# Running sums of logarithms and angles in a fused attention, expert and feed-forward kernel: exact fp32 products against products of numbers split in two parts

## The reference, cut to what matters

```python
mag = np.sqrt(a_re * a_re + a_im * a_im)
scale = np.minimum(mag, 0.999) / (mag + 1e-06)
a_re_n, a_im_n = (a_re * scale, a_im * scale)
for t in range(S):
    ar, ai = (a_re_n[:, :, t, :, None], a_im_n[:, :, t, :, None])
    new_re = ar * S_re - ai * S_im
    new_im = ar * S_im + ai * S_re
    kv = np.einsum('bhd,bhe->bhde', k[:, :, t], v[:, :, t])
    S_re, S_im = (new_re + kv, new_im)
    y[:, :, t] = np.einsum('bhd,bhde->bhe', q[:, :, t], S_re)
```

## Time and profile before

| what | value |
|---|---|
| median of 3 runs | 857.96 us (855.4 to 858.24) |
| the profiled execution | 854.9 us |
| its span, first to last instruction | 853.1 us |
| granted TensorE clock over the span | 0.996 of full speed |
| PE busy | 834.0 us, 98% |
| DVE, ACT, POOL busy | 362.0, 343.4, 158.8 us |

### The profile page before, as it was taken

How to read it: one execution, slowest core, us unless ns; L and a number is a source line. 1 busy time by engine, 2 the same in 40 slices (tenths; PEclk the granted TensorE clock), 3 DMA queues, 4 the chain that set the end, 5 groups by cost and what they waited for, 6 DMA issues and landing times.

```text
span 853.1 us, 13184 instructions
## 1 busy us (share of the span) xinstructions
PE 834.0 (98%) x5174; PEld 744.4 (87%) x5174; DVE 362.0 (42%) x677; ACT 343.4 (40%) x636; POOL 158.8 (19%) x196
## 2 busy tenths in 40 slices
PE   8899999999998899999999999999999999999997
PEld 6578888888897799999998998999999999999997
DVE  1588888889685333333322222132132132132112
ACT  6888988898653121111113222222222222222221
POOL 3111212622514124456200001001001001001001
PEclk9999999999999899999999999999999999999999
DMA  9999798586433689889600001001001001001001
GB/s 170 153 179 273 95 141 118 99 122 86 119 135 131 183 224 240 211 229 260 220 1 1 1 0 38 1 1 38 1 0 38 1 1 38 1 1 37 1 1 39
DMA packets 174998, 77.33 MB, mean 91 GB/s; under 512 B 152424, under 2 KB 168136, under 8 KB 174928
## 3 DMA queue, kind: packets, MB, share of 16 engines
q1 hardware_dynamic: 170000, 60.55, 35.2%
q0 software_dynamic: 4928, 15.84, 6.8%
HBM read 60.81 MB, written 15.59 MB: 90 GB/s over the span
## 4 chain that ended last, share of the span: by engine, by line
PE 90%; ACT 3%; issue 2%; DVE 2%; DMA 2%; POOL 1%; another core or an unknown queue 1%; SPq 0%; DVEq 0%; POOLq 0%; ACTq 0%
PE f_pU L1790 23%; PE f_pO L1796 23%; PE e_pH L1483 9%; PE e_pY L1499 9%; PE sc L572 5%; PE kvp L586 3%; PE yp L604 3%; PE yp L606 3%; PE sc L622 2%; PE tq L554 2%; PE tk L559 2%; PE cs L529 2%; PE cs L542 1%; PE cs L543 1%; DMA ring<-in_a_im 1%
## 5 line engine op out<-in xcount | busy, mean ns | idle before, releaser
L1790 PE MATMUL f_pU<-f_xT,wi 128*128 128x512 f32 x864 | 215.1, 395 | 0.8 <-DVE f_xT L1731 0.8
L1796 PE MATMUL f_pO<-wo,gT 128*128 128x384 f32 x1152 | 213.8, 336 | 0.0
L1796 PEld LDWEIGHTS f_pO<-wo,gT 128*128 128x128 f32 x1152 | 202.6, 188 | 7.5
L1790 PEld LDWEIGHTS f_pU<-f_xT,wi 128*128 128x128 f32 x864 | 161.3, 188 | 32.5 <-DVE f_xT L1731 1.2
L1747 DVE TENSOR_TENSOR gT<-g,gT 128x512 fp32r<-128x512 f32 x96 | 66.5, 693 | 286.5 <-ACT gT L1774 279.4
L1769 ACT ACTIVATE g<-f_pU 128x512 f32<-128x512 f32 x96 | 57.5, 599 | 298.2 <-PE f_pU L1790 298.2
L1737 POOL DMA_INDIRECT out<-o,row_of x24 | 24.1, 1005 | 413.3 <-DVE o L1758 406.9
L1483 PE MATMUL e_pH<-e_xT,ring 128*128 128x224 f32 x384 | 74.3, 353 | 0.7 <-DVE e_xT L1624 0.6
L1499 PE MATMUL e_pY<-hT,ring 128*128 128x224 f32 x384 | 74.1, 353 | 0.0
L1483 PEld LDWEIGHTS e_pH<-e_xT,ring 128*128 128x128 f32 x384 | 72.4, 190 | 1.0 <-issue 0.8
L1499 PEld LDWEIGHTS e_pY<-hT,ring 128*128 128x128 f32 x384 | 72.1, 190 | 0.0
(11 more groups left out here) (188 smaller groups left out, 981.6 us busy)
## 6 DMA issues: line engine op xcount, KB each, us to landing
ring<-in_moe_w SPq DMA_DIRECT2D x16, 1536.0 KB, 10.4
ring<-in_a_re SPq DMA_DIRECT2D x8, 576.0 KB, 8.6
ring<-in_a_im SPq DMA_DIRECT2D x8, 576.0 KB, 8.9
ring<-in_q SPq DMA_DIRECT2D x8, 576.0 KB, 7.8
ring<-in_k SPq DMA_DIRECT2D x8, 576.0 KB, 8.5
vraw<-in_v SPq DMA_DIRECT2D x8, 576.0 KB, 7.1
xs<-zero SPq DMA_DIRECT2D x9, 343.9 KB, 8.0
part<-in_moe_w_in POOLq DMA_DIRECT2D x12, 256.0 KB, 7.7
```

The lines of the kernel that those rows point to most:

```text
L1790: mm = pe.matmul(pU[f % 2][:, :], wi[:, pw, c, f * 128:(f + 1) * 128], xT[b % 2][:, px, c, :], start=(k == 1), stop=(k == NK * len(TERMS)))
L1796: mm = pe.matmul(pO[t][:, 0:DM], gT[f % GB][:, pg, t * 128:(t + 1) * 128], wo[:, pw, f, :], start=(f == 0 and k == 0), stop=(f == NF - 1 a ...
```

## The change

It makes both running sums, for the groups 1 to 7, from numbers split into two fp32r parts. POOL does the splitting. The parts are:

- `split(g, what, j)` on POOL: a cast of a piece (128 x 384) of `LM` or `AT` to fp32r, then the difference to the exact number, also as fp32r. The results go to one of two buffers `two`, in turn. It waits until the product that read this buffer before is done.
- `sum_l(g, j)` becomes two fp32r products with the same weights `tri_r`. `sum_phi(g, j)` becomes two fp32r products and one in fp32 with `PRE` and a matrix of ones.
- Since `tri_r` has plain ones, POOL first multiplies all of `AT` by 1/2pi (one instruction of 1152 columns, `share_done`).
- A piece is now a pair of chunks of all four heads, so that piece 0 of the angles needs `PRE` only for chunk 1, which is `AT` of chunk 0: its fp32 product has 192 columns. `PRE` has four chunks in place of six, made in four additions.
- In the feed-forward layer, the products of the first two blocks f = 0 and f = 1 are interleaved by chunk (`up_two`).

```diff
+            def split(g, what, j):
+                if not 1 <= g < G:
+                    return
+                i = nth(g, what, j)
+                hi, lo = two[i % 2][:, 0], two[i % 2][:, 1]
+                if j == 2:
+                    pool.wait_ge(s[("sum_l", "sum_phi")[what]], NPC * g + 1)
+                elif what == 1:
+                    pool.wait_ge(s["sum_l"], NPC * g + 2 + j)
+                elif g > 1:
+                    pool.wait_ge(s["sum_phi"], NPC * (g - 1) + 2 + j)
+                if what == 0:
+                    x = LM[:, :].rearrange("p (h c d) -> p h c d", h=HG, d=D)
+                    pool.wait_ge(s["l_done"], g + 1)
+                else:
+                    x = AT
+                    pool.wait_ge(s["share_done"], g)
+                x = x[:, :, CP * j:CP * (j + 1), :].rearrange("p h c d -> p h (c d)")
+                pool.tensor_copy(hi, x).then_inc(s["hi_done"], 1)
+                pool.wait_ge(s["hi_done"], i + 1)
+                pool.tensor_tensor(lo, x, hi, ALU.subtract).then_inc(s["two_done"], 1)
...
             for p in periods():
+                split(p + 1, 1, 2)
+                split(p + 2, 0, 0)
+                split(p + 2, 0, 1)
                 if here(p + 2):
                     prefix(p + 2)
...
                 if p in (3, 5, 7):
                     routing.scatter(pool, s, p // 2 - 1, xs, tile_paced if p == G - 1 else tile_here)
+                split(p + 2, 0, 2)
+                split(p + 2, 1, 0)
+                split(p + 2, 1, 1)
                 if p in (2, 4, 6):
                     routing.run(pool, s, p // 2 - 1)
...
+            def sum_two(g, what, j, last):
+                i = nth(g, what, j)
+                for k in range(2):
+                    mm = pe.matmul(cs[(NPC * what + j) % 2][:, 0:PW], tri_r[:, :],
+                                   two[i % 2][:, k].rearrange("p h e -> p (h e)"), start=(k == 0), stop=(last and k == 1))
+                return mm
...
             def sum_l(g, j):
-                pe.wait_ge(s["l_done"], g + 1)
+                if g == 0:
+                    pe.wait_ge(s["l_done"], 1)
+                else:
+                    pe.wait_ge(s["two_done"], nth(g, 0, j) + 1)
...
-                pe.matmul(bank, ptri[:, :], at[:, j * PW:(j + 1) * PW], start=True, stop=False)
-                pe.matmul(bank, pone[:, :], pre[:, j * PW:(j + 1) * PW], start=False, stop=True)\
-                    .then_inc(s["sum_phi"], 1)
+                    pe.wait_ge(s["two_done"], nth(g, 1, j) + 1)
+                    sum_two(g, 1, j, False)
+                whole = pone[:, :] if g == 0 else routing.ones[:, :]
+                if j == 0:
+                    mm = pe.matmul(bank(NPC + j)[:, :, D:2 * D], whole, AT[:, :, 0, :], start=False, stop=True)
+                else:
+                    mm = pe.matmul(bank(NPC + j), whole, PRE[:, :, CP * (j - 1):CP * j, :].rearrange("p h c d -> p h (c d)"),
+                                   start=False, stop=True)
+                mm.then_inc(s["sum_phi"], 1)
...
+            def up_two():
+                for c in range(NK - 1):
+                    up_block(0, c)
+                up_block(1, 0)
+                up_block(0, NK - 1)
+                for c in range(1, NK):
+                    up_block(1, c)
```

More of the change, by code:

```diff
@@ L278, in attention @@
     EPS = 1e-6
+    TURN = float(np.float32(0.5 / np.pi))
     B, H, S, D = q.shape
@@ L331, in attention @@
         AT = sb("AT", [128, HG, NC, D])
-        PRE = sb("PRE", [128, HG, NC, D])
+        PRE = sb("PRE", [128, HG, NC - 2, D])
         back_w = sb("back_w", [128, 2 * PAIRS, TW])
@@ L347, in attention @@
         YT = [sb(f"YT{i}", [128, PAIRS, C]) for i in range(2)]
+        tri_r = sb("tri_r", [128, C], mybir.dt.float32r)
+        two = [sb(f"two{i}", [128, 2, HG, PW // HG], mybir.dt.float32r) for i in range(2)]
         ONE, HPI, RND, LEPS = (cst[:, i:i + 1] for i in range(4))
@@ L381, in flat, with bank, nth @@
             return t.rearrange("p r d -> p (r d)")
+        CP = NC // NPC
         def piece(t, j):
-            return t[:, j * PW:(j + 1) * PW]
+            return t[:, :].rearrange("p (h c e) -> p h c e", h=HG, e=D)[:, :, CP * j:CP * (j + 1), :]\
+                .rearrange("p h c e -> p h (c e)")
+        def bank(j):
+            return cs[j % 2][:, 0:PW].rearrange("p (h e) -> p h e", h=HG)
+        def nth(g, what, j):
+            return 2 * NPC * (g - 1) + NPC * what + j
         def periods():
@@ L465, in gpsimd @@
                                pattern=[[1, C]], channel_multiplier=-1)
-            pool.memset(PRE[:, :, 0, :], 0.0)
             pool.memset(zero[:, :], 0.0)
@@ L528, in sum_l @@
                     pe.wait_ge(s["f_done"], NPC * g + 1)
-                pe.matmul(cs[j % 2][:, 0:PW], tri[:, :], piece(LM, j), start=True, stop=True).then_inc(s["sum_l"], 1)
+                if g == 0:
+                    mm = pe.matmul(bank(j), tri[:, :], piece(LM, j), start=True, stop=True)
+                else:
+                    mm = sum_two(g, 0, j, True)
+                mm.then_inc(s["sum_l"], 1)
             def sum_phi(g, j):
@@ L533, in sum_phi @@
                     return
-                at, pre = (t[:, :, :, :].rearrange("p h c d -> p (h c d)") for t in (AT, PRE))
                 pe.wait_ge(s["at_done"], g + 1)
-                pe.wait_ge(s["pre_done"], (NC - 1) * (g + 1))
+                if j > 0:
+                    pe.wait_ge(s["pre_done"], (NC - 2) * g + CP * j)
                 if j < 2:
@@ L734, in decays @@
                     act.wait_ge(s["fend_out"], 16 * g)
-                act.activation(piece(FD, j), cs[j % 2][:, 0:PW], ACT.Exp, scale=0.5)
-                act.activation(piece(FI, j), cs[j % 2][:, 0:PW], ACT.Exp, scale=-0.5).then_inc(s["f_done"], 1)
+                act.activation(piece(FD, j), bank(j), ACT.Exp, scale=0.5)
+                act.activation(piece(FI, j), bank(j), ACT.Exp, scale=-0.5).then_inc(s["f_done"], 1)
             def turns(g, j):
@@ L741, in turns @@
                     act.wait_ge(s["back_done"], g)
-                act.activation(piece(NN, j), cs[(NPC + j) % 2][:, 0:PW], ACT.Identity, bias=RND)\
+                act.activation(piece(NN, j), bank(NPC + j), ACT.Identity, bias=RND)\
                     .then_inc(s["rnd_done"], 1)
@@ L1792, in up, with up_block @@
                 mm.then_inc(s["up_done"], 1)
+            def up_block(f, c):
+                pe.wait_ge(e_s["part_lo"], c + 1)
+                pe.wait_ge(s["x_hi"], c + 1)
+                for k, (pw, px) in enumerate(TERMS):
+                    if px == 1:
+                        pe.wait_ge(s["x_out"], c + 1)
+                    mm = pe.matmul(pU[f][:, :], wi[:, pw, c, f * 128:(f + 1) * 128], xT[0][:, px, c, :],
+                                   start=(c == 0 and k == 0), stop=(c == NK - 1 and k == 2))
+                if c == NK - 1:
+                    mm.then_inc(s["up_done"], 1)
+            def up_two():
[5 more added lines that the diff above has]
+                    up_block(1, c)
             def down(b, f, t):
```

34 lines of the change are left out of this document (23 added, 11 removed).

## The result

The changed kernel takes 909.88 us (907.03 to 911.6, six runs), before 858.14 us in the same session: a ratio of 1.0608 (1.0583 to 1.0633), 52 us slower. Forecast were 875.5 us and a range from 856 to 892. The direction was right, the size was a third of what was measured.

The account below looks back on a forecast made before the run. PE, busy 98% of the span, was taken as the bound. Savings of 14.5 us against waits of 3.0, 10.2, 16.2 and 2.5 gave +17.4 us on the median 857.96, say 875.5 us, range 856 to 892.

Parts of the forecast that it names:

- The places: PE waits for POOL's splits: 1.5 us at plain seams, 5.1 at run seams, 8.1 at scatter seams, 2.5 at the start.
- The feed-forward layer: Interleaved blocks fill PE's 0.81 us wait for the third chunk with products that had to come anyway, saving 0.8 us.
- The blocks of 96 columns: Strided accesses of ACT and DVE with the same element counts, costed at nothing because both engines have slack once PE stands.
- the forecast's sign: Whole kernel: slower by more than 0.3% had chance 0.82, within it 0.07, faster 0.11.
- 3.0 + 10.2 + 16.2 + 2.5: PE's waits in us: periods 0 and 1, two seams with run, two seams with scatter, and the start.
- the cast's line: POOL's cast cost by columns, 0.617 us for 512 and 0.826 for 768; it priced the scaling at 1.14 us.
- What PE saves: Running sums in fp32r pairs of 0.37 us: 1.96 us a group, 13.7 us in seven groups.
- The one-hot seams: Periods 2 and 4: six one-hot additions ahead of split(g, 1, 2) on POOL, 5.1 us each, 10.2 together.
- the same chain: POOL's four splits at a seam, needed by sum_phi(g, 2); the one-hot additions lengthen it by 2.5 to 4.8 us, taken as 3.6.
- Rival 2: DVE loses the shared ports to POOL, making scores late; periods 0 to 5 cost 1 to 2 us more each: 884 us, chance 0.2.

Follow-up runs that it names:

- the version on ACT: Changed kernel with scatters and one-hot sums moved behind split(g, 1, 2) on POOL, and the angles scaled by ACT: 878.45 us, ratio 1.0254.
- the run of the pairs: Changed kernel without splits, scaling and fp32r products of the sums; chunk pairs and interleaved feed-forward blocks stay: 852.31 us, ratio 0.9962.
- the better order: Changed kernel with the scatters of periods 3 and 5 and the one-hot sums moved behind split(g, 1, 2) on POOL: 886.94 us, ratio 1.0393.
- The products alone: Changed kernel with only the first two pieces split and no scaling, PE multiplying what lies in the buffers without waiting: 848.03 us, ratio 0.9935.
- The ports alone: Kernel before, plus 42 POOL splits of the same size at the same places, of data and into buffers nobody reads: 863.29 us, ratio 1.0089.

## Why the prediction was wrong

**What held.** The places. PE waits for POOL's split behind the scatter in periods 3 and 5 (9.25 and 7.95 us, forecast 7.3). A split undisturbed is 1.5 us. In the version on ACT three seams have 2.65 us of waits for splits and three others one wait of 2.44 to 2.58 (two of these ended by DVE), against 1.5, with a bound of 3.3. The feed-forward layer gave 1.1 us for 0.8. The blocks of 96 columns, costed at nothing, cost nothing that can be seen (the run of the pairs). That a period's POOL work would run into DVE's ports was the argument for the forecast's sign.

**The sum, term by term.** For the attention the prediction had -13.7 us of PE's work and +31.9 of waits (3.0 + 10.2 + 16.2 + 2.5), and nothing else. The table above has -12.3 of work, +41.5 of waits and +26.7 of lost clock. So the largest error is the term that the sum put at nothing, the clock; the waits were 9.6 us too small. The scaling has a part in both.

**The cost that was wrong: "The scaling of `AT` (1152 columns, one input) goes by the cast's line: 1.14".** It is 3.12 us, 2.7 ns a column against the cast's 0.82; nothing in the trace of before had this instruction on POOL, and the sum kept no bound on it from the other side. By the line of the two-input differences (2.1 ns a column, 1.82 us for 768) it would have been 2.6. It was costed only as lead time for the splits. What it costs besides is DVE's time, which the sum did not have: 18.0 us between the runs with and without it in the better order, 24.5 in the changed kernel, both from single profiles, and 11.9 by the ratios against the scaling on ACT. In the sum it had 1.2 us at three places, 3.6.

**The term that was left out: the clock.** The prediction priced a wait of PE at its length. Behind the 9.25 us stand 8 us at half clock; behind 1.53 us stand 4 us at 0.59. Filling two waits with dead work gave 5.3 us back. That the splits and the scaling cost more together than by themselves fits this, for by themselves they lose 0.0 and 3.0 us to the clock; it was not tested apart. Moving the scatters gave 18.4 us for a forecast of 16.2, but the two waits were 17.2 us and the clock came on top, while other waits took their place: that the two numbers are close is luck.

**The saving that was too large: "What PE saves", 13.7 us in the attention.** The products alone are worth 5.6 us with the 1.1 of the feed-forward layer in it. A pair in its place takes 0.45 us, not the 0.37 of a long row of such products: with it the working gives 10.3, and PE's busy time fell by 10.5. Of these, 4.3 came back as waits. The text had costed both engines "at nothing" because they would have slack as soon as PE stands; where PE does not stand, they had none.

**The one-hot seams** were forecast at 10.2 us; moving them gave 0.5 us by the ratios, 3.5 us at the end of their interval, and 4.7 by the two profiles. The step that failed is that the sums add their length "to the same chain", with nothing else beside it: the chain through DVE to `FR` is nearly as long. PE waited 2.71 and 3.30 us, and still 1.85 and 2.24 with the sums moved.

**The sum, made again from the runs** (in us of 856): products -5.6; splits in the better order with the scaling on ACT +27.3 (1.0254 - 0.9935); the scaling on POOL instead +11.9 (1.0393 - 1.0254); the scatter ahead of the splits +18.4 (1.0608 - 1.0393). Together +52.0, as it must be, since each is the difference of two neighbours; in another order of the steps the shares could be others. By the ends of the attention the 27.3 are 21.1 for the splits and 9.0 for ACT's scaling (288.90 and 297.91), 2.8 more than by the ratios, which is the scatter of single profiles. The ports alone are 7.6 us (5.6 by the profile). The 21.1 are 13.1 of waiting and 8.5 of clock; how much of the waiting is due to there being only two buffers was not tested.

Rival 2, DVE as the loser of the ports, with 884 us and 0.2, was nearer than the forecast. Its mechanism is the one seen (L1007, KT, the scores), but its price for the clock was missing too.

The Trainium skill has the lock in "SBUF — State Buffer" (its sections on the two separate sides and on who interferes with whom): whichever of the two starts first keeps the shared ports for its whole instruction. The traces agree from the other side than the prediction looked: DVE's 0.35 us product that starts 0.2 us behind POOL's scaling takes 2.90 and ends with it. The Trainium skill, "GPSIMD Engine Reference" (section 3.1), has about 2.6 cycles for each element of a two-input addition on GpSimd against one on DVE; at the 1.2 GHz of its section 1 that is 2.2 ns, an estimate. The differences here took 2.1 ns a column, which agrees, and the scaling with one input was slower still, 2.7.

## What to carry to other kernels

Where PE is full and fed by two nearly full engines, do not price a wait at its length. Here 41.5 us of added waits came with 26.7 us of lost clock; a single wait cost nothing more (2.71 us at 165.13) or about as much again (1.53 us, and 0.41 of the 4.2 us behind it). Look at which queue the producer stands in (scatters ahead of it), and at which of several chains ends a wait: where DVE's was nearly as long, clearing POOL's gave little. Work that is moved to an idle POOL is not free: it takes DVE's ports, and an instruction that the trace has never shown on POOL needs a price bounded from the slow side. Measure the ceiling first: the products with nearly no splitting gave 0.65%, and 0.38% of it came without any split numbers.

## What the runs showed of the hardware

- POOL's multiplication of 1152 fp32 columns by a constant takes 3.12 us, in the changed kernel and on an unused tile alike; its cast of 384 columns to fp32r 0.50 and its difference 0.99 us.
- A DVE product of 192 columns that starts 0.2 us after such a multiplication ends with it: 2.90 us in place of 0.35. With the multiplication cut in three it took 0.52, but the three pieces took 4.31 us beside DVE's products in place of 3.5 (3 x 1.16), and the time stayed.
- PE behind a wait of 1.53 us: 0.59 of its clock over 4.2 us; behind 1.39 us (at 146.07): 0.50 from 147.2 to 153.2; behind 9.25 us: 0.50 over 8.0 us; but behind 0.41, 0.77, 1.41, 2.19 and 2.71 us: 1.00.
- Two fp32r products of 384 columns between fp32 ones take 0.45 us, in a long row of their kind 0.37.
